# Where VectorE looks for experts with too many rows: six small operations moved behind the work on expert 0's second tile

## The reference, cut to what matters

```python
h = x @ w_in                                   # 1536 x 384 @ 384 x 2048
g = np.where(h > 0.0, h, np.exp(np.minimum(h, 0.0)) - 1.0)
x = g @ w_out                                  # 2048 -> 384

logits = x @ w_gate                            # 8 experts
expert_idx = np.argmax(logits, axis=1)
gate_w = probs[np.arange(N), expert_idx]
# each token takes the next free row of its expert, up to capacity = 384 rows
h = np.maximum(np.einsum('ecd,edf->ecf', disp, w1), 0.0)
y = np.einsum('ecf,efd->ecd', h, w2)
out[i] = gate_w[i] * y[expert_idx[i], pos[i]]  # zero where the row did not fit
```

## Time and profile before

| | us |
|---|---|
| median of 3 runs | 433.55 |
| lowest, highest | 432.45, 434.67 |
| the profiled execution, own time | 433.79 |
| its span in the profile | 432.1 |
| TensorE busy in it | 413.7 (96%) |
| VectorE busy in it | 248.5 (58%) |
| GpSimd busy in it | 234.1 (54%) |
| mean granted clock of TensorE | 0.994 of full |

### The profile page before, as it was taken

How to read it: one execution, slowest core, us unless ns; L and a number is a source line. 1 busy time by engine, 2 the same in 40 slices (tenths; PEclk the granted TensorE clock), 3 DMA queues, 4 the chain that set the end, 5 groups by cost and what they waited for, 6 DMA issues and landing times.

```text
span 432.1 us, 9134 instructions
## 1 busy us (share of the span) xinstructions
PE 413.7 (96%) x3549; PEld 395.6 (92%) x3549; DVE 248.5 (58%) x595; ACT 182.1 (42%) x387; POOL 234.1 (54%) x242
## 2 busy tenths in 40 slices
PE   8779999999999999999999999996999999999994
PEld 8669789999999999999999998996999999999994
DVE  7868746564576456645664476786456355454521
ACT  4356534423333333333333455452456454564520
POOL 1878746647675856685563334164062744726431
PEclk9999999999999999999999999998999999999999
DMA  7999959304030403020008001724545837539000
GB/s 244 402 388 385 358 181 370 128 1 150 2 114 2 150 2 115 2 103 2 1 20 329 2 0 49 292 82 159 198 160 197 308 108 295 207 147 339 22 32 26
DMA packets 18504, 65.55 MB, mean 152 GB/s; under 512 B 2059, under 2 KB 11573, under 8 KB 16288
## 3 DMA queue, kind: packets, MB, share of 16 engines
q1 hardware_dynamic: 16672, 60.26, 38.6%
q0 software_dynamic: 1792, 4.73, 2.9%
HBM read 52.56 MB, written 13.21 MB: 152 GB/s over the span
## 4 chain that ended last, share of the span: by engine, by line
PE 70%; DVE 11%; issue 5%; DMA 5%; POOL 4%; ACT 3%; SPq 0%; POOLq 0%; DVEq 0%; ACTq 0%
PE bank L1278 21%; PE bank L1280 20%; PE bank L1279 19%; DMA xrow<-slots 2%; ACT elu L792 2%; DVE elu L1104 2%; PE bank L1296 2%; DVE wd_lo L990 1%; DMA rkt<-rkt 1%; DMA nat<-nat 1%; DVE wd_lo L1194 1%; POOL g_lo L653 1%; DVE wd_lo L995 1%; PE bank L1324 1%; PE bank L1360 1%
## 5 line engine op out<-in xcount | busy, mean ns | idle before, releaser
L653 POOL TENSOR_TENSOR g_lo<-elu,g_hi 128x256 fp32r<-128x256 f32 x95 | 74.2, 782 | 95.7 <-ACT g_hi L794 94.9
L1278 PE MATMUL bank<-xt,wd_hi 128*128 128x256 f32 x288 | 81.9, 284 | 4.2 <-DVE elu L1107 2.3
L792 ACT ACTIVATE elu<-elu 128x256 f32<-128x256 f32 x96 | 40.1, 418 | 105.5 <-DVE elu L1104 105.3
L1280 PE MATMUL bank<-xt,wd_lo 128*128 128x256 f32 x288 | 81.2, 282 | 0.0
L1279 PE MATMUL bank<-xt,wd_hi 128*128 128x256 f32 x288 | 81.2, 282 | 0.0
L1278 PE MATMUL bank<-wd_hi,g_hi 128*128 128x392 f32 (+1 forms) x192 | 68.2, 355 | 0.3 <-ACT x2row L764 0.3
L1107 DVE SCALAR_TENSOR_TENSOR elu<-elu,bank 128x256 f32<-128x256 f32 x96 | 40.4, 421 | 47.4 <-ACT elu L792 47.4
L1104 DVE TENSOR_SCALAR elu<-bank 128x256 f32<-128x256 f32 x96 | 40.3, 420 | 47.3 <-PE bank L1280 46.6
L1280 PE MATMUL bank<-wd_hi,g_lo 128*128 128x392 f32 (+1 forms) x192 | 65.1, 339 | 0.0
L1279 PE MATMUL bank<-wd_lo,g_hi 128*128 128x392 f32 (+1 forms) x192 | 65.1, 339 | 0.0
L1278 PEld LDWEIGHTS bank<-xt,wd_hi 128*128 128x128 f32 x288 | 54.5, 189 | 6.5 <-DVE elu L1107 3.7
(11 more groups left out here) (210 smaller groups left out, 945.6 us busy)
## 6 DMA issues: line engine op xcount, KB each, us to landing
we_raw<-wexp SPq DMA_DIRECT2D x8, 1536.0 KB, 7.1
wd_raw<-wexp SPq DMA_DIRECT2D x8, 1536.0 KB, 8.2
nat<-nat SPq DMA_DIRECT2D x10, 672.0 KB, 4.5
rkt<-rkt SPq DMA_DIRECT2D x12, 512.0 KB, 6.7
xrow<-slots SPq DMA_DIRECT2D x16, 193.0 KB, 7.1
wd_raw<-win SPq DMA_DIRECT2D x4, 768.0 KB, 8.8
wd_raw<-wout SPq DMA_DIRECT2D x4, 768.0 KB, 11.1
wo_tr<-wouttr SPq DMA_DIRECT2D x1, 3072.0 KB, 16.9
```

What stands on the lines that cost most here:

```text
L653: nc.gpsimd.tensor_tensor(g_lo[:, f % 4, :], elu[:, f % 2, :], g_hi[:, f % 4, :].bitcast(F32), ALU.subtract).then_inc(s_glo, 1)
L792: nc.scalar.activation(elu[:, f % 2, :], elu[:, f % 2, :], ACT.Exp).then_inc(s_exp, 1)
L1278: mm(dst, w_hi, x_hi, start=start, stop=False)
L1280: return mm(dst, w_lo, x_hi, start=False, stop=stop)
```

## The change

The six operations go from their place behind `gated(0, ...)` to one behind `tokens_of(1, ...)`, before VectorE waits for the end of expert 0's second tile. Nothing else is touched.

```diff
@@ -1195,12 +1195,6 @@
                                 ALU.subtract).then_inc(s_elo1[1], 1)
             dve.wait_ge(s_y0, 1)
             gated(0, ps_y[0][:, 0:DM])
-            link(V.tensor_copy(part3[:, 0, :], ps_tot))
-            link(V.tensor_tensor(part3[:, 1, 0:1], part3[:, 0, 0:1], early0[:, :], ALU.subtract))
-            link(V.tensor_tensor(part3[:, 1, 1:2], part3[:, 1, 0:1], early0[:, :], ALU.max))
-            link(V.tensor_scalar_add(part3[:, 0, 0:1], part3[:, 1, 1:2], float(SN - C)))
-            link(V.tensor_reduce(col3[:, 1, 0:1], part3[:, 0, :], AXX, ALU.max))
-            V.tensor_copy(n_over[:, :], col3[:, 1, 0:1]).then_inc(s_over, 1)
 
             def expert_x(i, r):
@@ -1241,6 +1235,12 @@
                 tile_lo(b, ps_ht[1], s_gehi, s_gelo, ET // 2)
             expert_x(0, 1)
             tokens_of(1, s_tok[0])
+            link(V.tensor_copy(part3[:, 0, :], ps_tot))
+            link(V.tensor_tensor(part3[:, 1, 0:1], part3[:, 0, 0:1], early0[:, :], ALU.subtract))
+            link(V.tensor_tensor(part3[:, 1, 1:2], part3[:, 1, 0:1], early0[:, :], ALU.max))
+            link(V.tensor_scalar_add(part3[:, 0, 0:1], part3[:, 1, 1:2], float(SN - C)))
+            link(V.tensor_reduce(col3[:, 1, 0:1], part3[:, 0, :], AXX, ALU.max))
+            V.tensor_copy(n_over[:, :], col3[:, 1, 0:1]).then_inc(s_over, 1)
             dve.wait_ge(s_fc2e, ET)
             gated(1, ps_y[0][:, 0:DM])
             expert(0, 1, True)
```

## The result

| | before | after |
|---|---|---|
| median of the runs, us | 433.58 (4 runs) | 428.99 (4 runs) |
| lowest, highest | 432.45, 434.67 | 428.51, 430.16 |
| ratio, 95% interval | | 0.9898 [0.9866, 0.9931] |
| the profiled execution, own time | 433.79 | 430.16 |
| its span | 432.1 | 428.3 |

The change made the kernel 4.6 us faster, 1.0% (by the interval 0.7 to 1.3%). The forecast was 429.0. The two profiled executions differ by 3.63 us only. The table by stretch shows why: the one of after had a slow stretch near its start, which the change does not touch. These are its first columns in the same form as the earlier trace rows, first the kernel before, then the changed one.

A forecast was written before the change was run, and what follows sets the result against it. TensorE, busy 413.7 of 432.1 us, was taken as the bound; 3.28 us of earlier start plus 1.35 of clock made 4.63 off 433.79, 429.16, or 428.92 from the median; forecast 429.0 us, range 427.7 to 431.1.

The forecast's parts named there:

- Release of line 1158: VectorE starts line 1158 about 0.05 us after TensorE delivers, so TensorE's transposes of half 1 start 3.29 us earlier.
- From the last first-layer matmul to `tile_fc2`: In expert 0's second tile, `tile_fc2` begins at 294.46 instead of 297.74, a gain of 3.28 us.
- The low part of half 1: It ends at 296.16 instead of 299.44, in time by 0.4 us for `tile_fc2`, which wants it halfway.
- The clock: TensorE keeps full clock in `tile_fc2` of expert 0's second tile: 4.27 instead of 5.62 us, 1.35 us gained.
- The six in the new place: Behind `tokens_of(1)` the six operations take 1.0 us in all, hidden in VectorE's wait for `tile_fc2`: cost 0.
- The cover: VectorE's 3.13 us wait before `gated(1)`, shortened by 1.35, hides the six moved operations with 0.6 us left.
- Other queues: Loads elsewhere stay in time; the one not tied to TensorE, expert 2's first-layer weights, has 1.8 us to spare.
- The sum: Earlier `tile_fc2` start and full clock together gain 3.28 + 1.35 = 4.63 us, which lasts to the kernel's end.
- A: Rival: the clock still falls to 0.50 for `tile_fc2`, only 3.28 us gained, 430.5 us; chance 0.08.
- B: Rival: the six operations are slow by themselves, 4.60 us in the new place; gain 2.7, time 431.1; chance 0.05.
- C: Rival: a load not tied to TensorE becomes late and the whole gain is given back, 433.6 us; chance 0.07.
- D: Rival: the six delay `gated(1)` and the load of expert 2's rows, making the kernel slower, 436.6 us; chance 0.03.

The follow-up runs named there:

- filler experiment: The kernel before with 14 extra matmuls filling TensorE's 3.4 us wait before the transposes of half 1: 432.41 us, ratio 0.9962.
- the changed kernel again: The changed kernel run once more, unaltered, as the mark for the other experiments: 428.87 us, ratio 0.9886 to the kernel before.

## Why the prediction was right

Point by point, by its own steps, against the profile after:

- *Release of line 1158.* Taken as 0.05 us behind TensorE; it was 294.07 - (293.64 + 0.39) = 0.04.
- *From the last first-layer matmul to `tile_fc2`.* Worked out as 294.46 - 292.60 = 1.86 us; it was 1.86. The small wait on the low part was there as described: `tile_fc2` begins 295.50 - (294.68 + 0.68) = 0.14 us behind the low part's end, the distance of before.
- *The low part of half 1.* Forecast 3.56 us behind the zero, at 296.16; it ended 296.94 - 293.64 = 3.30 behind it. It was 0.26 earlier because ScalarE's copy in front of it follows transposes that were themselves faster at full clock. That only adds margin.
- *The clock.* 1.35 us forecast, 5.62 - 4.26 = 1.36 measured. The filler experiment shows it as a term of its own. That the clock would always fall in the kernel before was taken for granted; at least 2 of its 37 executions in the experiments were spared.
- *The six in the new place.* 1.0 us forecast, 298.82 + 0.15 - 297.85 = 1.12 measured, with 0.19 to 0.20 from start to start rather than 0.18. Cost 0 forecast and, against the run without them, 0 measured. The cover left was 0.99 us instead of 0.6. That nothing of GpSimd's would stand beside the six was not quite so: its scatter of tile 0 ran from 297.06 to 298.06, and the six, early by the 0.26 above, began at 297.85. The first of them took 0.16 us all the same.
- *Other queues.* ScalarE's first use of expert 2's weights follows its eviction at the distance of before, 0.28 us (306.86 to 307.14 there), so the one untied load was in time. ScalarE's timeline after:

```profile
303.27 0.39 ACT L856 ACTIVATE ge_hi<-bank 128x256 fp32r<-128x256 f32 x1 [0.82 <-PE bank L1280]
303.55 1.04 ACT L861 CAST we_hi<-we_raw 128x1024 fp32r<-128x1024 f32 x1
```

- *The sum.* Expert 1 began 299.76 - 293.64 = 6.12 us behind the zero, against 303.36 - 292.60 = 10.76: 4.64 us gained, 4.63 forecast. It reached the end: 4.59 by the medians of the first runs, 4.77 by the second.
- *The rivals.* A would have needed a fall of the clock behind a gap of 0.12 us; in the profiled executions it did not fall behind 0.67 or 1.76 either. B's premise, that the operations are long by themselves, fell with the 0.16 us. C and D did not happen: from 240 us to the end TensorE has no wait above 0.3 us left.

Some of it was right for thinner reasons than it looks. That GpSimd's work and not the operations' own length was the cause rested on two coinciding ends, and the 1.0 us for the six leaned on it; it was shown only afterwards. The cover was worked out beforehand, but the place matters: behind line 1158, a few instructions earlier, the same six cost nearly everything. And that the median came within 0.01 us of 429.0 is luck: the four executions spread from 428.51 to 430.16, and the interval allows gains of 3.0 to 5.8 us.

## What to carry to other kernels

When an operation on one element takes microseconds, compare its end with the ends of GpSimd's operations: here the cure could be the place, an input in PSUM or as a pointer scalar, or a GpSimd that starts later, and all three gave the same within the noise, 4.5 to 4.8 us. Work that nobody waits for soon belongs where its engine waits anyway, and its price there is that of the next thing behind it, so check each consumer behind the new place and not only the one that was freed. A stall of TensorE of about 3 us is to be counted with the slow matmuls behind it, 1.3 us more in most executions of this kernel.

## What the runs showed of the hardware that was not expected

- The hold goes both ways: VectorE's and GpSimd's three weight differences took 5.70 and 9.09 us when they met, and 3.48 and 7.08 when they did not. VectorE's third one alone went from 3.43 to 1.22 us. The profile shows no wait for it, since the held time is counted as busy time.
- TensorE's granted clock after idle stretches, in the profiled executions: still 1.00 after single gaps of 0.67 and 1.76 us; 0.50 after 2.94 and 3.40 us, where the matmuls then ran slow for about 3 us. It is not the same in every execution of one kernel: after 2.94 us the clock did not fall in at least 3 of 12, by their times and mean clocks.
- The clock near the start of the execution differs from run to run in the same code. From 12 to 24 us it was 1.00 in the profile before, 0.86 in the one of the changed kernel again and 0.72 in the first one of the changed kernel, and everything behind it stood 1.04 us later in the last than in the first. Two single profiles could not have told a change of 1 us apart.
